# First four hidden tiles from raw float32 tokens and weights, with a new order of work for all engines up to the second token chunk

## The reference

```
k_p, v_p = means of k and v over groups of 8 tokens
attn = softmax(q @ k_p.T / 8);  x = attn @ v_p           # (4608, 512)
h = x @ w_in1                                            # (4608, 2048)
g = where(h >= 1, h, where(h <= -1, 0, (h + 1)**2 / 4))
x2 = g @ w_out1                                          # (4608, 512)
out = relu(x2 @ w_in2)**2 @ w_out2
```

## Time and profile before

| | us |
|---|---|
| median of 3 runs | 1581.32 (1580.9 to 1581.43) |
| profiled execution | 1581.02 |
| its span, first to last instruction | 1579.2 |
| TensorE busy | 1560.1 (99%) |
| VectorE / ScalarE / GpSimd busy | 1150.0 / 862.1 / 244.9 |
| mean granted TensorE clock | 0.999 |

### The profile page before, as it was taken

How to read it: one execution, slowest core, us unless ns; L and a number is a source line. 1 busy time by engine, 2 the same in 40 slices (tenths; PEclk the granted TensorE clock), 3 DMA queues, 4 the chain that set the end, 5 groups by cost and what they waited for, 6 DMA issues and landing times.

```text
span 1579.2 us, 25435 instructions
## 1 busy us (share of the span) xinstructions
PE 1560.1 (99%) x9130; PEld 1545.8 (98%) x9130; DVE 1150.0 (73%) x1894; ACT 862.1 (55%) x1616; POOL 244.9 (16%) x353
## 2 busy tenths in 40 slices
PE   6999999999999999999999999999999999999999
PEld 5999999999999999999999999999999999999999
DVE  7777667667666777767869766667667986876874
ACT  4767678777767634444445654444456643443442
POOL 7536438726500000000000000000000000000000
PEclk9999999999999999999999999999999999999999
DMA  9376569557637553344344642442448645245231
GB/s 283 107 227 228 180 213 331 207 195 241 210 118 221 180 171 119 121 161 136 105 160 132 251 144 102 160 145 96 160 154 284 194 155 190 71 147 189 91 115 40
DMA packets 174461, 265.92 MB, mean 168 GB/s; under 512 B 15616, under 2 KB 152832, under 8 KB 174336
## 3 DMA queue, kind: packets, MB, share of 16 engines
q1 hardware_dynamic: 174336, 264.30, 50.2%
HBM read 157.29 MB, written 106.95 MB: 167 GB/s over the span
## 4 chain that ended last, share of the span: by engine, by line
PE 94%; DVE 3%; ACT 1%; issue 1%; DMA 0%; POOL 0%; DVEq 0%; ACTq 0%; POOLq 0%
PE bank L787 42%; PE bank L677 24%; PE bank L810 22%; PE bank L640 2%; PE bank L651 1%; DVE gf L1200 1%; PE bank L666 1%; DVE b L1193 1%; PE bank L669 1%; PE bank L667 1%; PE bank L668 1%; DVE f_lo L1168 0%; PE bank L655 0%; ACT pT_rest L864 0%; ACT wi_hi L882 0%
## 5 line engine op out<-in xcount | busy, mean ns | idle before, releaser
L787 PE MATMUL bank<-gf,f_hi 128*128 128x384 f32 x2688 | 681.8, 334 | 0.4 <-DVE u_b L1210 0.3
L787 PEld LDWEIGHTS bank<-gf,f_hi 128*128 128x128 f32 x2688 | 484.9, 188 | 1.2 <-DVE u_b L1210 0.8
L787 PE MATMUL bank<-gf,f_lo 128*128 128x384 f32 x1344 | 448.9, 334 | 0.0
L911 ACT ACTIVATE gf<-b 128x768 fp32r<-128x768 f32 x336 | 278.6, 845 | 262.7 <-PE bank L787 177.0
L1200 DVE TENSOR_TENSOR gf<-b,gf 128x768 fp32r<-128x768 f32 x336 | 314.2, 951 | 43.4 <-ACT gf L911 43.4
L810 PE MATMUL bank<-xf,w_hi 128*128 128x384 f32 x1344 | 341.1, 334 | 0.0
L677 PE MATMUL bank<-x_hi,wi_hi 128*128 128x384 f32 x768 | 265.7, 346 | 1.5 <-DVE g_st L1281 0.8
L677 PE MATMUL bank<-x_hi,wi_lo 128*128 128x384 f32 x768 | 257.6, 335 | 0.0
L677 PE MATMUL bank<-x_lo,wi_hi 128*128 128x384 f32 x768 | 257.6, 335 | 0.0
L787 PEld LDWEIGHTS bank<-gf,f_lo 128*128 128x128 f32 x1344 | 252.3, 188 | 0.0
L810 PEld LDWEIGHTS bank<-xf,w_hi 128*128 128x128 f32 x1344 | 242.8, 188 | 0.0
(11 more groups left out here) (96 smaller groups left out, 1472.4 us busy)
## 6 DMA issues: line engine op xcount, KB each, us to landing
b<-g_dram SPq DMA_DIRECT2D x192, 384.0 KB, 4.1
g_dram<-g_st SPq DMA_DIRECT2D x192, 192.0 KB, 2.2
g_dram<-c_st SPq DMA_DIRECT2D x192, 192.0 KB, 1.9
s_dram<-su_s SPq DMA_DIRECT2D x24, 512.0 KB, 2.8
k_raw<-k SPq DMA_DIRECT2D x32, 288.0 KB, 3.5
q_sb<-q SPq DMA_DIRECT2D x48, 192.0 KB, 2.8
y_dram<-o_st SPq DMA_DIRECT2D x48, 192.0 KB, 1.9
x_raw<-y_dram SPq DMA_DIRECT2D x24, 384.0 KB, 5.1
```

Source lines behind the costliest of these rows:

```text
L787: last = mm(dst[:, 0:H], w[:, 2 * i + kt, cols], x[:, half, kt, :], start=q_ < 3 and i == 0 and kt == 0 and h == 0, stop=q_ >= 4 and i == ...
L911: copy(gf[layer][r % GRING][:, 0], unit_source(n)[:, 2 * i:2 * i + 2, :], ACT.Copy).then_inc(gf_hi, 1)
```

## The change

- Slots 0 to 3 (`FIRST` = 4) are made with one float32 matmul per block, of the unsplit weights `wi_raw` and a new unsplit copy `x_first` of the tokens, instead of three of split operands. Slot 3 uses a bank of the scores. The split tokens of chunk 0 are made from `x_first`, for slots 4 to 15. Weights 0 to 3 are split later, for chunk 1; the order of the splits is 4 to 15, then 0 to 3.
- pT_hi, pT_lo and pT_rest have two buffers each. `REST_APART` becomes 8.
- The rest of the values is loaded as three DMAs of 16 rows instead of one of 96 rows, which held the same 16 rows three times between zeros.
- The first addition over the values (`fold`) is a step apart, put ahead of the low part of the pair before.
- `keep_warm(n)` adds n transposes of the identity whose result nothing reads: 15, 10 and 6.
- The lists of all engines are rewritten up to the second chunk, and pairs 4 to 6 are placed one slot later.

SP's loads now come in this order: k0 q0 k1 v0 q1 k2 v1 q2 k3, weights 0 to 3, q3 v2 k4, weight 4, q4, weight 5, v3, weight 6, k5, weight 7, q5, weight 8, v4, weights 9 to 11, v5, weights 12 to 15.

The core of the diff (renamings, the matching counters and the store of the rest buffers are left out):

```diff
-    REST_APART = HP + 1
+    FIRST, WI_DVE = 4, 2
+    REST_APART = 2 * HP
...
-            first = {4: 0, 5: 3, 6: 6, 7: 9}
+            first = {4: 1, 5: 4, 6: 7, 7: 9}
+        def h_bank(g):
+            return h_ps[g] if g < FIRST - 1 else s_ps[1] if g == FIRST - 1 else h_ps[(g - FIRST) % HRING]
+        def h_before(g):
+            return g - HRING if g < FIRST + HRING else g - HRING + 1
+        def wi_count(j):
+            return (j - FIRST) % NF + 1
...
         @block.sync
...
-                sp.dma_start(v_raw[n][0:REST_ROWS, 1], v_rest[m // HP, m % HP]).then_inc(v_in[n], 16)
+                for row in range(0, REST_ROWS, 32):
+                    sp.dma_start(v_raw[n][row:row + REST, 1], v_rest[m // HP, m % HP]).then_inc(v_in[n], 16)
...
+            sp.wait_ge(zeros_made, 4 + VRAW)
             load_v(0)
...
         @block.gpsimd
...
+            fold(0)
             values(0)
+            for m in range(HP):
+                if m + 2 <= HP:
+                    spread_keys(m + 2)
+                fold(m + 1)
                 values_low(m)
+                values(m + 1)
+            weights_low(6)
+            values_low(4)
+            weights_low(7)
...
+            pool.wait_ge(h_full, FIRST)
+            for j in range(FIRST):
+                weights_low(j)
...
         @block.tensor
...
             def scores(a):
...
+                if a == HP + 1:
+                    pe.wait_ge(g_made, FIRST)
...
-                pe.wait_ge(g_made, g - HRING + 1)
+                pe.wait_ge(g_made, h_before(g))
...
+            def first_hidden(kt, slots):
+                pe.wait_ge(x_first_ready, kt + 1)
+                for g in slots:
                     if kt == 0:
+                        pe.wait_ge(weight_in[g], 16)
+                        if g == FIRST - 1:
+                            pe.wait_ge(s_prob, HP)
+                    last = mm(h_bank(g)[:, 0:H], wi_raw[g][:, kt * P:(kt + 1) * P], x_first[:, kt, :],
+                              start=kt == 0, stop=kt == KT - 1)
+                    if kt == KT - 1:
+                        last.then_inc(h_full, 1)
+            def keep_warm(count):
+                for _ in range(count):
+                    tr(h_ps[0][:, 0:P], ident[:, :], ident[:, :])
...
+            keep_warm(15)
             scores(0)
+            keep_warm(10)
             scores(1)
             transposes(0)
+            keep_warm(6)
             scores(2)
+            transposes(1)
             values(0)
-            transposes(1)
             scores(3)
+            first_hidden(0, range(FIRST - 1))
+            transposes(2)
             values(1)
-            transposes(2)
+            first_hidden(1, range(FIRST - 1))
             scores(4)
-            first_hidden(0)
+            for kt in range(2):
+                first_hidden(kt, (FIRST - 1,))
+            transposes(3)
             values(2)
-            transposes(3)
-            first_hidden(1)
             values(3)
-            first_hidden(2)
-            first_hidden(3)
-            for g in range(HRING, SLOTS):
+            for kt in range(2, KT):
+                first_hidden(kt, range(FIRST))
+            for g in range(FIRST, SLOTS):
                 slot(g)
...
         @block.scalar
...
             def probabilities(a):
                 act.wait_ge(t_full, a + 1)
-                if a:
-                    act.wait_ge(pv_full, a)
+                if a >= 2:
+                    act.wait_ge(pv_full, a - 1)
...
+            def tokens_first(a):
+                act.wait_ge(pv_full, a + 1)
+                copy(x_first[:, a, :], o_ps[:, 0:H], ACT.Copy).then_inc(x_first_ready, 1)
...
             exps(0)
-            weights_high(0)
+            exps(1)
             values_high(0)
-            exps(1)
             for a in range(HP):
                 probabilities(a)
+                for j in ((), (4, 5), (), (6,))[a]:
+                    weights_high(j)
+                if a < 2:
+                    exps(a + 2)
+                tokens_first(a)
                 values_high(a + 1)
-                for j in ((1,), (2,), (3,), (4, 5))[a]:
-                    weights_high(j)
                 tokens_high(a)
-                if a == 3:
-                    weights_high(6)
-                if a + 2 <= HP:
-                    exps(a + 2)
+                if a == 2:
+                    exps(4)
+            weights_high(7)
+            weights_high(8)
             for g in range(SLOTS):
                 slot(g)
-                if g + 7 < NF:
-                    weights_high(g + 7)
+                if g + 9 < NF:
+                    weights_high(g + 9)
+                if 8 <= g < 8 + FIRST:
+                    weights_high(g - 8)
...
         @block.vector
...
             keys(0)
+            for one in pT_rest:
+                vec.memset(one[:, :].bitcast(F32), 0.0).then_inc(mask_made, 1)
+            below(0)
             keys(1)
-            below(0)
             normal(0)
             below(1)
             keys(2)
             for a in range(HP):
                 if a + 1 < HP:
                     normal(a + 1)
+                if a == 1:
+                    tokens_low(0)
+                if a == 2:
+                    tokens_low(1)
+                if a == 3:
+                    weights_low(4)
                 probabilities_low(a)
                 if a + 2 <= HP:
                     below(a + 2)
-                if a + 3 < 6:
+                if a + 3 <= 5:
                     keys(a + 3)
-                if a == 3:
-                    weights_low(4)
-                tokens_low(a)
-                for j in ((0,), (1, 2), (3,), ())[a]:
-                    weights_low(j)
+            tokens_low(2)
+            weights_low(5)
+            tokens_low(3)
             normal(4)
```

More of the change, by code:

```diff
@@ L593, in slot @@
                         spread_keys(m)
+                        fold(m)
                         values(m)
@@ L604, in _ @@
             spread_keys(1)
-            pool.wait_ge(mask_made, 5)
+            pool.wait_ge(mask_made, 4)
+            fold(0)
             values(0)
[L607 to L611, removed]
-                values_low(m)
-            for m, more in ((5, (5, 6)), (6, (7, 8)), (7, (11, 12))):
-                spread_keys(m)
-                for j in more:
-                    weights_low(j)
[L617 to L622, removed]
+            for m in range(HP):
+                if m + 2 <= HP:
+                    spread_keys(m + 2)
+                fold(m + 1)
+                values_low(m)
+                values(m + 1)
+            weights_low(6)
+            values_low(4)
+            weights_low(7)
+            spread_keys(5)
+            fold(5)
+            values(5)
+            weights_low(8)
+            values_low(5)
+            weights_low(9)
+            spread_keys(6)
+            fold(6)
+            values(6)
+            weights_low(10)
+            weights_low(11)
+            values_low(6)
+            spread_keys(7)
+            fold(7)
+            values(7)
+            weights_low(12)
+            values_low(7)
+            for j in range(13, NF):
+                weights_low(j)
+            pool.wait_ge(h_full, FIRST)
+            for j in range(FIRST):
+                weights_low(j)
             for g in range(SLOTS):
@@ L665, in values @@
                     cols, vh, vl = slice(n0, n1), v_hi[m % KRING], v_lo[m % KRING]
[L666 to L669, removed]
+                    mm(o_ps[:, cols], vh[:, 0, :], hi[:, cols], start=True, stop=False)
+                    mm(o_ps[:, cols], vh[:, 0, :], lo[:, cols], start=False, stop=False)
+                    mm(o_ps[:, cols], vl[:, :], hi[:, cols], start=False, stop=False)
+                    last = mm(o_ps[:, cols], vh[0:REST_ROWS, 1, :], rows[:, cols], start=False, stop=True)
                 last.then_inc(pv_full, 1)
@@ L1155, in tokens_low @@
                 dve.wait_ge(x_hi_ready, a + 1)
[L1156 removed]
+                raw = o_ps[:, 0:H] if c else x_first[:, hp, :]
+                vec.tensor_tensor(x_lo[c % 2][:, hp, :], raw, x_hi[c % 2][:, hp, :].bitcast(F32),
                                   ALU.subtract).then_inc(x_ready, 1)
             def weights_low(j):
[L1160 removed]
+                dve.wait_ge(wi_hi_ready, wi_count(j))
                 vec.tensor_tensor(wi_lo[j][:, :], wi_raw[j][:, :], wi_hi[j][:, :].bitcast(F32), ALU.subtract)\
@@ L1280, in slot @@
                     h = g_st[g % GST]
-                    vec.scalar_tensor_tensor(h[:, :], h[:, :], 1.0, h_ps[g % HRING][:, 0:H], ALU.min, ALU.max)\
+                    vec.scalar_tensor_tensor(h[:, :], h[:, :], 1.0, h_bank(g)[:, 0:H], ALU.min, ALU.max)\
                         .then_inc(g_made, 1)
-                if g == 2:
-                    keys(6)
+                for m, at_slot in ((6, 4), (7, 8)):
+                    if g == at_slot:
+                        keys(m)
                 for n, at_slot in enumerate((17, 16, 15, 14, 9, 8)):
```

(5 more changed lines are left out.)

100 lines of the change are left out of this document (53 added, 47 removed).

## The result

Over 22 runs of each the changed kernel takes 1584.24 us (1582.76 to 1586.37), the kernel before 1581.40 (1580.9 to 1581.93): 2.8 us slower, ratio 1.0019 with a 95% interval of 1.0012 to 1.0025. The profiled execution took 1583.86 us with a span of 1582.1. TensorE is busy for 1565.2 us. The runs also spread over 3.6 us, where those of before spread over 1.0.

A forecast was written before the change was run, and what follows sets the result against it. TensorE was taken to bound the kernel. -0.3 us with an ideal clock and +2.3 us for the clock gave +2.0 us: 1583.0 against the profiled 1581.02, stated as 1583.3 us, range 1578.0 to 1587.0.

The forecast's parts named there:

- lists as laid out and a fall of the clock: The forecast case, from the start to slot 16: +2.0 us, chance 0.50.
- What bounds: TensorE, busy 1560.1 of 1579.2 us: the change can only win or lose in the beginning, nearly all in the first slice.
- Raw blocks: Float32 blocks of slots 0 to 3 on TensorE: 0.325 us a record, 1.7 us more than the three matmuls replaced.
- The tie: TensorE around pair 3's values: 5.2 us of raw blocks remain after them, against about 5.4 us done before them.
- Start of values(3): Values of pair 3 on TensorE: start at 33.0 us, 1.0 us earlier, after 4.1 us idle behind ScalarE's list.
- x_lo beside GpSimd: VectorE's x_lo(0) and x_lo(1) beside GpSimd: at the upper end twice their 0.56 us, adding 0.7 us; not taken.
- The wait of scores(5): TensorE waits 2.0 us, to 43.8 us, until slot 3 leaves the score bank; the 1.0 us gain is spent here.
- Slots 5 to 15: From there to slot 16: dearer transposes against the 0.58 us wait at pair 6; stretch counted -0.3 us, between -1.0 and +0.7.
- The clock: Clock falls on the 4.1 us gap before values(3): taken at +2.3 us, between 0 and 2.6.
- The early clock failing: Rival 1, transposes(1) to values(1), 15 to 22 us: low clock adds +1.5 to +2 us, 1585.3; chance 0.17.
- Rival 2: ScalarE's list does not hold pair 3 back; values(3) at 29.5 us, clock stays, -3.5 us, 1577.8; chance 0.14.
- The loads of the rest rows: Rival 4: these loads come late and stop GpSimd's folds, +1.6 us over the forecast and more; chance 0.04.

The follow-up runs named there:

- e3: The changed kernel with the values' high part and transposed probabilities of pair 3 ahead of pair 2's token copy on ScalarE; 1579.04 us.
- e2b: The changed kernel with 30 transposes in the wait before values(3) and 14 in the wait before scores(5); 1581.84 us.
- e2c: The kernel of e2b run once more, for its trace; 1582.13 us.
- e11: e9 with keys(1) ahead of below(0) on VectorE again, as in the kernel before; 1578.65 us.
- e4: The changed kernel with ScalarE's weight splits of slots 0 to 2 moved behind slot 3; 1583.86 us.
- e6: e3 with weight splits 9 to 11 on ScalarE ahead of slot 0, and keys(7) on VectorE at slot 6 instead of 8; 1579.07 us.
- e10: e9 with REST_APART back at 5, so four transposes and six small copies for pairs 5 to 7; 1580.43 us.
- e7: e3 with the wait before scores(5) filled with 14 transposes; 1579.17 us.
- e1: The changed kernel without its 31 keep-warm transposes; 1586.45 us.
- e8: e6 with 9 transposes in the wait before transposes(1) and 5 in the wait before scores(3); 1578.5 us.
- e9: e8 with 10 transposes also in the wait before values(3); 1578.41 us.

## Why the prediction was right

The forecast was +2.0 us for the case of lists as laid out and a fall of the clock; measured are +2.8. The mechanism was the forecast one: ScalarE's order makes a wait of 4.1 us before values(3), the clock falls on it, and the raw blocks behind it pay (e3, e2b, e2c). That the number came so close is in part luck. Values(3) were put 0.7 us too late and the fall 0.7 us too dear, and these errors hid most of a second fall of 1.6 us that the sum did not have. Step by step:

- *What bounds.* Right: by slot 16 the spans are 2.6 of 2.9 us apart.
- *Raw blocks.* Right: 16 records in 5.33 us in e2c at the high clock, 0.33 us a record (0.325 forecast), and 6 in 2.10. The tie came out too: these blocks take 38.57 - 33.37 = 5.2 us, and what they replace took 41.12 - 34.81 = 6.3 in the kernel before, of which 0.8 were a wait. So the rival that the raw blocks cost the time is out.
- *Start of values(3).* Forecast 33.0 us after 4.1 us of wait; it was 32.34 after 4.12. The links were the ones named, with values(2) at 27.26 and ScalarE's 2.9 us behind them; e3 shows that ScalarE's order makes the gap. The 0.7 us too much were in the first links: scores(0) ended 0.7 us earlier because the clock was up by then, and the spread values of pair 0 came only 0.3 us after ScalarE was ready for them. The step still carries about half of what it is given: in e11 scores(1) start 1.0 us earlier and values(3) 0.5.
- *x_lo beside GpSimd.* x_lo(0) and x_lo(1) took 0.57 us, not double, so the upper end was not reached; GpSimd's v_lo, which ran beside them, took 0.78 and 0.77 us instead of 0.45. x_lo(2), at 32.31, took 1.46 us beside a GpSimd operation that had begun at 32.08, but no wait of TensorE hangs on it. So VectorE paid in one case of three, and GpSimd in the other two.
- *The wait of scores(5).* Forecast 2.0 us until 43.8; it was 1.70 until 44.72, later because the raw blocks had run at the low clock. e4 and e6 confirm its cause.
- *Slots 5 to 15.* The term was -0.3 us; without the second fall the stretch lost 0.2. The dearer transposes and the wait of 0.58 us at pair 6 nearly balance, as I had set them. What e10 measures is something else: in the new list, with its later pairs, the old value of REST_APART would cost 2.0 us. It is not a gain over the kernel before.
- *The clock.* One fall was forecast at 0 to 2.6 us, taken at 2.3, and measured at 1.64. (In the kernel before, the fall at 21.1 us came 0.3 us before the gap ended at 21.41, not after it, as the forecast says; the gap up to it was 1.8 us.) A second, behind the wait of scores(5), was not forecast at all, and took about 1.6 us more: from the mark to pair 9 are 37.03 us here and 79.80 - 44.37 = 35.43 in e2c. By the estimate from the mean clocks every run had one to three falls. This is the step by which the sum came out low: -1.66 (pair 3 earlier) + 1.64 (first fall) + 0.85 (the rest up to the mark, the wait in it) + 1.6 (second fall) + 0.2 (slots 5 to 16) = +2.6 us at slot 16.
- *Rivals.* The early clock failing: the profiles of e3, e4 and e6 show a low stretch between 15 and 21 us, so it happened in some executions. Its price, at values(3): from scores(1) to values(3) are 24.9 us in e4 and 23.7 in the changed kernel, 22.0 in e3 and 21.4 in e7, so 0.6 to 1.2 us where 1.5 to 2 were forecast. (The 2.2 us of e1 are another thing, the clock low from the start.) Rival 2 named ScalarE's list as what would have to give way: e3 made it give way, and won 5.2 us against the changed kernel where 5.5 (from +2.0 to -3.5) were forecast; against the kernel before that is -2.5, not -3.5, with values(3) at 30.7 and not 29.5. The loads of the rest rows were never waited for: GpSimd has no wait for a load in the first 60 us, where the kernel before had two of 1.5 us in total. The three small loads were not tried by themselves.

## What to carry to other kernels

A wait of TensorE costs what it lasts and, if the clock falls on it, up to 1.6 us more, which is paid behind it. It is paid only where TensorE itself is what the time waits for: in the kernel before the fall at 21 us stood ahead of another wait and was free. Before an engine's list is rewritten, ask of each copy what stands behind it in the same list: one token copy ahead of the probabilities that did not need it cost 5.2 us, with the falls of the clock that came with it. A wait that is removed uncovers the next one in the list, so the two are changed together. And when the clock differs from run to run, read the mean clock of all runs before taking the profiled one as typical.

## What the runs showed of the hardware

- Transposes of float32 raise the clock and hold it: in the one list of e6, e8 and e9, with 31, 45 and 55 of them in the waits, four of 11, eight of 10 and 11 of 11 runs read a mean of 1.00. The number alone is no guarantee: with 75 in e2c, in other waits, only three of 10 runs did, and with 31 in e3 eight of 11.
- The same wait does not always let the clock fall: 1.9 us before values(3) did so in e6's profile and not in e3's. Which it is changes from one execution to the next: the runs of the changed kernel read means of 0.997 to 0.999.
- A fall widens the spread of times only where nothing hides it. The 104 runs of the kernel before read 0.996 to 1.00 and lie within 1.4 us all together; the 22 of the changed kernel spread over 3.6, and the 11 of e9, all at 1.00, over 1.8.
